# First loads on two queues, the first pair's scores in whole fp32, and the order of the attention's drain, in a fused attention, feed-forward and routed-experts kernel

## The chip, the cores and the metric

The kernel runs on one core of one Trainium2 chip. The metric is the device time of one execution in microseconds (us); the median of several runs is compared.

## The reference

Three stages follow one another, and only the first and the beginning of the second are touched here.

```
attention, q, k, v: (4, 8, 576, 64)
    scores = q @ k^T / 8, block-causal mask (blocks of 64), softmax, @ v
feed-forward, x: (2304, 512), w_in: (512, 2048), w_out: (2048, 512)
    h = x @ w_in;  g = h if h > 0 else exp(h) - 1;  x = g @ w_out
experts, 8 of them, top one of a gate, rows with x @ w_skip > 0
    out = x + gate * (relu(x @ w1[e]) @ w2[e])
```

## The kernel before

The 32 heads are worked on as 16 pairs: the two heads of a pair have 64 columns each, and lie side by side on the 128 partitions. A pair's step on TensorE holds the scores of five row blocks (`scores(n, i, u)`, u = 0 to 4, into the PSUM tile `s_ps`), the transposes of the softmax's rows (`turn_pair`, `turn_head`, `turn_last`, `turn_corner`, into `t_ps`), the transposes of the next pair's q and k (`prep`, groups g = 0, 1, 2 of 4, 1 and 4 transposes), and the products with v (`values`, into `o_ps`). The pairs are software pipelined: while pair n is scored, pair n - 1 is turned and pair n - 2's products with v end. The order on each engine is written out by hand in `step`, and the engines meet only at semaphores.

All large products are made in three passes of a rounded type: each operand is split in a high and a low half (`qk_hi`, `qk_lo`; `wi_hi`, `wi_lo`; `xt_hi`, `xt_lo`; `wo_hi`, `wo_lo`), and high x high, low x high and high x low are added up. The scores of block u = 0 alone are made from the unsplit `qk_f` in plain fp32 (L587). ScalarE copies q and k out of PSUM into `qk_f` (`prep_copy`, L493 to L500); GpSimd splits them for the pairs 1 to 15, VectorE for pair 0 (L437, L439).

SyncE issues every plain load and store, in one queue. At the start it issues q, k of pair 0, q, k of pair 1, v of both, and so on, three DMAs each (L228 twice, L230). For each pair it also stores the 9 x 128 reciprocals of the row sums to DRAM (L250), loads them back spread over the partitions (`load_recips`, L257 and L260, four DMAs), and stores the pair's result, `attn_sb`, to `attn_t` (`store`, L244). VectorE multiplies the result by the spread reciprocals (`final`, L424) before that store.

The drain is what follows the last pair's step. TensorE turns block 3 of pair 15, ends pair 14's products, makes `hidden(0)` (the feed-forward's first h chunk, 12 matmuls with 384 columns), turns the reciprocals into `t_ps`, waits until ScalarE has copied them out, turns the last block, makes `hidden(1)` and then pair 15's products with v. After that the feed-forward's steps begin: `ff_hidden(0, f)`, 12 matmuls, and two chunks behind it `ff_output(0, f - 2)`, 9 matmuls with 512 columns. The output product of chunk f needs chunk f of w_out in both halves: SyncE loads it (L1048, 256 KB, into one of four buffers, waiting until GpSimd has made the low half of the chunk four before), ScalarE makes the high half (`wo_high`, L1576), GpSimd the low half (L1166). ScalarE's steps are in program order: `wo_high(f + 2)`, `exp(0, f)`, `g_hi(0, f - 1)`. GpSimd, after the low half of chunk 3, waits for the store of all pairs' results and writes constants (L1109 to L1125) before it makes the low half of chunk 4. The chunks 0 to 3 of w_out are loaded ahead of the last reciprocals, chunk 4 behind the last store, the others behind the loads of the next x block:

```
for f in range(WR, FC):
    load_wo(f)
    if f == WR:
        for stored in attend["stored"]:
            sp.wait_ge(stored, 16 * attend["pairs"] // 2)
        load_x(1)
        load_gates()
```

## Time and profile before

| | |
|---|---|
| Median of 3 runs | 828.46 us (827.02 to 831.72) |
| The profiled execution's own time | 828.58 us |
| Its span, first to last instruction | 826.8 us |
| TensorE matmuls busy | 797.1 us, 96% of the span |
| VectorE, ScalarE, GpSimd busy | 530.1, 341.4, 244.9 us |
| Attention and its drain | from the start to about 203 us |
| Feed-forward | to about 640 us, experts after it |

Times are read from the start of the span. "PEld" is TensorE's weight load, "SPq" the issuing of a DMA on SyncE, and the bracket at the end of a row of the timeline is the engine's idle time just before the instruction and what ended it. A matmul's row begins when it begins; rows overlap, since matmuls are pipelined.

### The profile page before, as it was taken

To read this page: it belongs to the slowest core of one execution; us is meant where nothing else is said; L and a number is where in the kernel's file an instruction comes from. 1 tells how busy PE (TensorE), PEld (TensorE's weight loads), DVE (VectorE), ACT (ScalarE), POOL (GpSimd) and SP (SyncE) were. 2 spreads that over 40 slices of the span, in tenths; PEclk is the share of its full clock that TensorE was granted. 3 is DMA by queue.
4 is the path that set the end of the run, shared out by engine and by line. 5 is a ranking of instruction groups with operands and counts; after the bars stand their busy time and mean duration, and the time that the engine had idled before them with its cause. 6 is when DMAs were issued, how large, how long until landed. Compare 5 with 4: busy or idle time off the path is not lost.

```text
span 826.8 us, 14738 instructions
## 1 busy us (share of the span) xinstructions
PE 797.1 (96%) x4618; PEld 663.0 (80%) x4619; DVE 530.1 (64%) x1294; ACT 341.4 (41%) x831; POOL 244.9 (30%) x240
## 2 busy tenths in 40 slices
PE   5999999999999999999999999999997999999995
PEld 3777777777889988888888898889875777887884
DVE  3777778775433587488478658734765799267342
ACT  3666666563442322222322232232443676256141
POOL 2667766675351021021012002000012313123111
PEclk9999999999999999999999999999998999999998
DMA  6355556644424201200110020050341799264000
GB/s 141 99 145 155 158 155 155 169 134 144 116 65 160 86 20 61 77 21 20 64 32 20 1 77 7 20 204 3 126 161 31 236 324 366 81 223 148 20 27 8
DMA packets 102912, 88.09 MB, mean 107 GB/s; under 512 B 66676, under 2 KB 78340, under 8 KB 102736
## 3 DMA queue, kind: packets, MB, share of 16 engines
q1 hardware_dynamic: 99808, 82.48, 32.4%
q0 software_dynamic: 3056, 5.00, 1.8%
q8 instruction: 26, 0.43, 0.2%
q14 instruction: 22, 0.18, 0.1%
HBM read 72.26 MB, written 18.34 MB: 110 GB/s over the span
## 4 chain that ended last, share of the span: by engine, by line
PE 74%; SPq 12%; DMA 4%; issue 4%; DVE 3%; ACT 1%; DVEq 1%; POOL 0%; POOLq 0%; ACTq 0%
PE h_ps L1686 11%; PE out_ps L1686 11%; PE h_ps L1687 11%; PE h_ps L1688 11%; PE out_ps L1688 11%; PE out_ps L1687 11%; SPq L228 4%; SPq L230 3%; DMA recip_rows<-r_rows 3%; SPq L260 2%; SPq L257 2%; PE t_ps L600 1%; PE o_ps L650 1%; PE out_ps L1822 1%; PE s_ps L592 1%
## 5 line engine op out<-in xcount | busy, mean ns | idle before, releaser
L1513 ACT ACTIVATE ex<-h_ps 128x384 f32<-128x384 f32 x96 | 47.1, 491 | 269.1 <-PE h_ps L1688 268.5
L1686 PE MATMUL h_ps<-xt_hi,wi_hi 128*128 128x384 f32 x384 | 131.9, 343 | 0.0
L1687 PE MATMUL h_ps<-xt_lo,wi_hi 128*128 128x384 f32 x384 | 129.9, 338 | 0.0
L1688 PE MATMUL h_ps<-xt_hi,wi_lo 128*128 128x384 f32 x384 | 129.9, 338 | 0.0
L1352 DVE TENSOR_SCALAR ex<-ex 128x384 f32<-128x384 f32 x96 | 36.9, 384 | 143.3 <-ACT ex L1513 142.2
L1686 PE MATMUL out_ps<-wo_hi,gt 128*128 128x512 f32 x288 | 114.8, 398 | 1.8 <-DVE gt L1345 1.8
L1688 PE MATMUL out_ps<-wo_hi,gt 128*128 128x512 f32 x288 | 114.0, 396 | 0.0
L1687 PE MATMUL out_ps<-wo_lo,gt 128*128 128x512 f32 x288 | 113.4, 394 | 0.0
L512 ACT ACTIVATE prob<-s_ps,negmax 128x128 f32<-128x128 f32 (+2 forms) x144 | 77.8, 548 | 63.9 <-DVE negmax L379 57.9
L1234 DVE CUSTOM_DVE_ANT_0 x2t<-x,w_raw 128x512 bf16<-128x512 f32 x108 | 82.8, 808 | 0.4
L1130 POOL TENSOR_TENSOR xt_lo<-x_raw,xt_hi 128x384 fp32r<-128x384 f32 x20 | 28.4, 1419 | 163.0 <-ACT xt_hi L1528 162.9
L1686 PEld LDWEIGHTS h_ps<-xt_hi,wi_hi 128*128 128x128 f32 x384 | 72.3, 188 | 3.4
L1687 PEld LDWEIGHTS h_ps<-xt_lo,wi_hi 128*128 128x128 f32 x384 | 72.3, 188 | 3.1
L1138 POOL DMA_INDIRECT route_table<-entry,slot x18 | 21.0, 1165 | 177.2 <-DVE slot L1313 160.9
L1688 PEld LDWEIGHTS h_ps<-xt_hi,wi_lo 128*128 128x128 f32 x384 | 72.2, 188 | 0.0
L379 DVE TENSOR_REDUCE negmax<-s_ps 128x2 f32<-128x256 f32 (+1 forms) x64 | 51.3, 823 | 21.5 <-PE s_ps L595 21.5
L1688 PEld LDWEIGHTS out_ps<-wo_hi,gt 128*128 128x128 f32 x288 | 54.2, 188 | 13.3
L1686 PEld LDWEIGHTS out_ps<-wo_hi,gt 128*128 128x128 f32 x288 | 54.1, 188 | 11.4 <-issue 2.4
L1687 PEld LDWEIGHTS out_ps<-wo_lo,gt 128*128 128x128 f32 x288 | 54.1, 188 | 8.8
L600 PE MATMUL t_ps<-ident,prob 128*128 128x128 f32 (+1 forms) x400 | 58.5, 284 | 1.6 <-DVE pt L403 0.7
L1355 DVE TENSOR_TENSOR ex<-h_ps,ex 128x384 f32<-128x384 f32 x96 | 53.5, 558 | 3.3
L600 PEld LDWEIGHTS t_ps<-ident,prob 128*128 128x128 f32 (+1 forms) x400 | 43.5, 141 | 13.8 <-issue 11.3
(174 smaller groups left out, 1629.8 us busy)
## 6 DMA issues: line engine op xcount, KB each, us to landing
w_raw<-in_moe_w_dram SPq DMA_DIRECT2D x56, 512.0 KB, 5.2
attn_t<-attn_sb SPq DMA_DIRECT2D x16, 288.0 KB, 2.2
x_raw<-attn_t SPq DMA_DIRECT2D x24, 192.0 KB, 2.4
out_dram<-x SPq DMA_DIRECT2D x18, 256.0 KB, 2.1
x_rows<-x SPq DMA_DIRECT2D x18, 256.0 KB, 2.5
raw_qk<-in_q_dram SPq DMA_DIRECT2D x32, 128.0 KB, 2.4
raw_qk<-in_k_dram SPq DMA_DIRECT2D x32, 128.0 KB, 2.4
v<-in_v_dram SPq DMA_DIRECT2D x32, 128.0 KB, 2.6
```

What stands on the lines that cost most here:

```text
L228: sp.dma_start(dst[:, 0:FULL, h, :], heads[h, 0:FULL * P, :] .rearrange("(t p) d -> p t d", p=P)).then_inc(landed, 16)
L379: dve.tensor_reduce(heads_cols(negmax, u), s_pair(u), AX_X, ALU.max, negate=True).then_inc(max_done, 1)
L512: act.activation(dst, src, ACT.Exp, bias=negmax[:, c:c + 1], accum_out=rowsum[i][:, c:c + 1]).then_inc(exp_done, 1)
L600: return pe.transpose(t_ps[0:src.shape[1], bank, at:at + P], src, ident[:, :])
L1130: pool.tensor_tensor(xtk(b % 2, 1, k), x_raw[k][:, :], xtk(b % 2, 0, k).bitcast(F32), ALU.subtract).then_inc(x_lo_done, 1)
L1234: ins = dve.tensor_tensor_reduce(dot_rows[:, ((E + 1) * t + e) % 2], x2[s][:, :], all_skip if e == E else all_gates[:, e, :], 1.0, 0.0, AL ...
L1352: dve.tensor_scalar(e, e, 1.0, -1.0, ALU.min, ALU.add).then_inc(em_done, 1)
L1355: dve.tensor_tensor(e, h_ps[:, f % 2, 0:NB], e, ALU.max).then_inc(g_done, 1)
L1513: act.activation(ex[:, f % 2], h_ps[:, f % 2, 0:NB], ACT.Exp).then_inc(ex_done, 1)
L1686: pe.matmul(dst, stat[0], mov[0], start=start, stop=False, skip_group_check=True)
L1687: pe.matmul(dst, stat[0], mov[1], start=False, stop=False, skip_group_check=True)
L1688: return pe.matmul(dst, stat[1], mov[0], start=False, stop=stop, skip_group_check=True)
```

## The change

Five edits:

- The loads of k for the pairs 0 and 1 are issued on ScalarE's queue, at its very beginning; those of q stay on SyncE's.
- Pair 0's three groups of transposes go to three PSUM banks (two of `t_ps`, one of `o_ps`) without a wait between them. VectorE copies the third group out, in place of ScalarE, and no longer splits pair 0.
- Pair 0's scores are made from the unsplit `qk_f` in plain fp32 in all five blocks.
- In the drain, `hidden(0)` comes before the turns of block 3; the last block and the corner are turned before the reciprocals, and these go to a free place in `s_ps` (`last_rows`). The turn of the last block waits for VectorE's copy of block 3 in place of ScalarE's copy of the reciprocals.
- Chunks 4 to 7 of w_out are issued after the last reciprocals' loads and ahead of the last store; the loads of the next x block and of the gates follow that store.

```
+    def load_q(eng, n, i):
+        load(eng, q, n, raw[i][:, 0], raw_tail[i][0:TAIL], qk_in[i])
+    def load_k(eng, n, i):
+        load(eng, k, n, raw[i][:, 1], raw_tail[i][TAIL:P], qk_in[i])
...
-        load_qk(0, 0)
-        load_qk(1, 1)
+        for i in range(2):
+            load_q(sp, i, i)
         load_v(0, 0)
...
-        load_wo()
+        first_wo()
         store_recips(PAIRS - 1, 1)
         store(PAIRS - 2, 0)
         load_recips(PAIRS - 1, 1)
+        next_wo()
         store(PAIRS - 1, 1)
...
-                pool.wait_ge(split_hi, 2 * n + part + 1)
+                pool.wait_ge(split_hi, 2 * (n - 1) + part + 1)
...
-        for part, (a, b) in enumerate(((Q, K), (K, QK))):
-            dve.wait_ge(prep_out, (1, 3)[part])
-            dve.tensor_copy(qk_hi[0][:, a:b], qk_f[0][:, a:b]).then_inc(split_hi, 1)
-            dve.wait_ge(split_hi, part + 1)
-            dve.tensor_tensor(qk_lo[0][:, a:b], qk_f[0][:, a:b], qk_hi[0][:, a:b].bitcast(F32),
-                              ALU.subtract).then_inc(split_lo, 1)
+        dve.wait_ge(prep_t, 3)
+        dve.tensor_copy(qk_f[0][:, K:K + FULL * P], o_ps[:, 0:BANK]).then_inc(split_lo, 2)
...
-        for g in range(3):
-            prep_copy(0, 0, g, (0, 1, 0)[g])
+        for i in range(2):
+            load_k(act, i, i)
+        for g in range(2):
+            prep_copy(0, 0, g, g)
...
+            whole = isinstance(n, int) and n == 0
             if u == 0:
                 wait(pe, exp_done, exps(n - 1, 3, 1))
                 wait(pe, split_lo, 2 * n + 2)
+                if whole:
+                    pe.wait_ge(prep_out, 3)
...
+                    if whole:
+                        last = pe.matmul(dst, qk_f[i][:, Q4:QK], qk_f[i][:, keys], start=True, stop=True)
+                        continue
...
-            if u == 0:
+            if u == 0 or whole:
...
         for g in range(3):
-            if g == 2:
-                pe.wait_ge(prep_out, 1)
-            prep(0, 0, g, (0, 1, 0)[g])
+            prep_into(0, 0, g, t_ps[:, g] if g < 2 else o_ps[:, 0:BANK])
...
+        pe.wait_ge(wi_lo_done, PAIRS)
+        pe.wait_ge(exp_done, exps(last[0], 3, 1))
+        hidden(0)
         for h in range(2):
             turn_head(last[0], 3, h)
         values(*older, 1)
-        pe.wait_ge(wi_lo_done, PAIRS)
-        hidden(0)
-        pe.wait_ge(turned, turns(last[0], 3, 1))
+        turn_last(last[0], turned, turns(last[0], 3, 1))
+        turn_corner(last[0])
         pe.wait_ge(rec_done, PAIRS)
-        turn_recips(last[0])
-        turn_last(last[0])
-        turn_corner(last[0])
+        turn_recips(last_rows)
         hidden(1)
...
-            attend["sync"](sp, first_wo)
-            for f in range(WR, FC):
+            attend["sync"](sp, first_wo, next_wo)
+            for stored in attend["stored"]:
+                sp.wait_ge(stored, 16 * attend["pairs"] // 2)
+            load_x(1)
+            load_gates()
+            for f in range(2 * WR, FC):
                 load_wo(f)
```

## Rows read from the trace of the kernel before

**Rows 1.** The page, the chain that ended last, shares by engine

```profile
PE 74%; SPq 12%; DMA 4%; issue 4%; DVE 3%; ACT 1%; DVEq 1%; POOL 0%; POOLq 0%; ACTq 0%
```

**Rows 2.** Busy time in a stretch (us, count) of PE, PEld, DVE, ACT, POOL; clock; DMA share; GB/s

```profile
68.20:79.40 11.20, 11.20 (x103) 8.21 (x99) 8.78 (x17) 7.22 (x25) 7.60 (x7) 1.00 0.60 156
```

**Rows 3.** The chain that ended last, the first loads: start, us, what

```profile
0.87 0.45 SPq L228
...
3.89 2.42 DMA raw_tail<-in_k_dram
```

**Rows 4.** Busy time in a stretch, columns as in Rows 2, first loads

```profile
2.00:4.00 2.00, 0.00 (x0) 0.00 (x0) 0.06 (x1) 1.28 (x1) 0.15 (x2) 1.00 0.65 148
```

**Rows 5.** Timeline of the start, PE, ACT: start, us, engine, line, what, idle before

```profile
2.23 1.28 ACT L493 ACT_TABLE_LOAD   x1 [2.08 <-POOL qk_f L318]
...
6.45 1.08 PE L559 MATMUL t_ps<-ident,raw_qk 128*128 128x128 f32 x4 [6.45 <-DMA raw_tail<-in_k_dram]
...
7.32 0.42 PE L559 MATMUL t_ps<-ident,raw_tail 128*128 128x128 f32 x1
...
11.50 0.80 PE L587 MATMUL s_ps<-qk_f 64*128 64x128 f32 x4 [2.17 <-DVE qk_lo L439]
...
12.09 0.27 PE L595 MATMUL s_ps<-mask_row,half_row 64*128 64x64 bf16 x2
```

**Rows 6.** The page, the costliest groups: a DMA issued by another engine than SyncE

```profile
L1138 POOL DMA_INDIRECT route_table<-entry,slot x18 | 21.0, 1165 | 177.2 <-DVE slot L1313 160.9
```

**Rows 7.** Timeline, pair 0's step and the beginning of pair 1's, PE

```profile
16.59 1.12 PE L559 MATMUL t_ps<-ident,raw_qk 128*128 128x128 f32 x4 [0.76 <-ACT qk_f L493]
...
18.23 0.63 PE L592 MATMUL s_ps<-qk_hi,qk_lo 64*128 64x512 f32 x2
...
18.66 0.63 PE L592 MATMUL s_ps<-qk_lo,qk_hi 64*128 64x512 f32 x2
...
23.23 0.49 PE L587 MATMUL s_ps<-qk_f 64*128 64x128 f32 x4
```

**Rows 8.** The line L424 on VectorE: what it waited for (us, times)

```profile
  DMA r_sb<-recip_rows: 2.4, 1
```

**Rows 9.** Timeline of the drain, POOL, PE, DVE, SP

```profile
191.25 0.99 POOL L358 TENSOR_TENSOR xt_lo<-x_raw,xt_hi 128x384 fp32r<-128x384 f32 x1
...
192.13 1.09 PE L600 MATMUL t_ps<-ident,prob 128*128 128x128 f32 x8 [0.41 <-DVE pt L397]
...
196.51 0.27 PE L600 MATMUL t_ps<-ident,recip 128*9 128x128 f32 x1
...
197.23 0.74 PE L600 MATMUL t_ps<-ident,prob 128*128 128x128 f32 x5 [0.45 <-ACT r_rows L525]
...
197.89 0.69 DVE L403 COPY pt<-t_ps 128x512 f32<-128x512 f32 x1 [2.73 <-PE t_ps L600]
...
200.13 0.60 SPq L260 DMA_DIRECT2D r_sb<-recip_rows  x1
...
202.96 0.76 DVE L424 TENSOR_TENSOR attn_sb<-o_ps,r_sb 128x576 f32<-128x576 f32 x1 [0.92 <-PE o_ps L650]
```

**Rows 10.** DMA issues from 185 to 240: count, KB each, median us to landing

```profile
w_raw<-in_moe_w_out_dram SPq DMA_DIRECT2D x15, 256.0 KB, 3.1
...
r_sb<-recip_rows SPq DMA_DIRECT2D x4, 16.0 KB, 2.7
```

**Rows 11.** Timeline of the feed-forward's first steps, SP, ACT, POOL, PE

```profile
203.75 0.34 SPq L244 DMA_DIRECT2D attn_t<-attn_sb  x1
...
206.87 0.63 ACT L1576 ACTIVATE wo_hi<-w_raw 128x512 fp32r<-128x512 f32 x1 [5.87 <-DMA w_raw<-in_moe_w_out_dram]
...
207.81 1.29 POOL L1166 TENSOR_TENSOR wo_lo<-w_raw,wo_hi 128x512 fp32r<-128x512 f32 x1
...
210.52 0.47 PE L1686 MATMUL out_ps<-wo_hi,gt 128*128 128x512 f32 x1 [1.11 <-DVE gt L1345]
...
215.61 0.47 PE L1686 MATMUL out_ps<-wo_hi,gt 128*128 128x512 f32 x1 [0.66 <-DVE gt L1345]
```

More of the change, by code:

```diff
@@ L221, in heads_cols, with load, sync @@
         return t[:, 0:2 * FULL].rearrange("p (h u) -> p h u", h=2)[:, :, u]
[L223 to L230 removed]
+    last_rows = s_ps[0:COLS, 2 * BANK:2 * BANK + P]
+    def load(eng, t, n, dst, tail, landed):
+        heads = t.rearrange("b h s d -> (b h) s d")[bass.ds(2 * n, 2)]
+        for h in range(2):
+            eng.dma_start(dst[:, 0:FULL, h, :], heads[h, 0:FULL * P, :]
+                          .rearrange("(t p) d -> p t d", p=P)).then_inc(landed, 16)
+        eng.dma_start(tail, heads[:, FULL * P:S, :].rearrange("h s d -> s h d")).then_inc(landed, 16)
+    def load_q(eng, n, i):
+        load(eng, q, n, raw[i][:, 0], raw_tail[i][0:TAIL], qk_in[i])
+    def load_k(eng, n, i):
+        load(eng, k, n, raw[i][:, 1], raw_tail[i][TAIL:P], qk_in[i])
+    def sync(sp, first_wo, next_wo):
         def load_qk(n, i):
             wait(sp, prep_t, 3 * (n - 1))
[L235 to L236 removed]
+            load_q(sp, n, i)
+            load_k(sp, n, i)
         def load_v(n, i):
             wait(sp, pv_done, n - 1)
[L240 removed]
+            load(sp, v, n, vb[i], vb[i][0:TAIL, FULL, :, :], v_in[i])
         def store(n, i):
@@ L500, in prep_copy @@
                 act.activation(qk_f[i][:, K + FULL * P:Q4], src[:, TAIL:P], ACT.Copy)\
-                   .then_inc(prep_out, 1)
+                   .then_inc(prep_out, 2 if isinstance(n, int) and n == 0 else 1)
         def exp(n, i, u):
@@ L538, in step @@
             if past:
-                recip_rows(past[0])
+                recip_rows(past[0], t_ps[0:COLS, 1, R0:R0 + P])
             if now:
@@ L549, in scalar, with prep_into @@
         wo_high()
-        recip_rows(PAIRS - 1)
+        recip_rows(PAIRS - 1, last_rows)
     def tensor(pe, hidden):
         def prep(n, i, g, bank):
+            prep_into(n, i, g, t_ps[:, bank])
+        def prep_into(n, i, g, dst):
             if g == 0:
@@ L558, in prep @@
             for c, tile in enumerate(tiles):
-                last = pe.transpose(t_ps[:, bank, c * P:(c + 1) * P],
+                last = pe.transpose(dst[:, c * P:(c + 1) * P],
                                     tile.rearrange("p h d -> p (h d)"), ident[:, :])
@@ L626, in turn_head, with turn_last @@
             last.then_inc(pt_done, 1)
-        def turn_last(n):
+        def turn_last(n, ready, value):
             wait(pe, exp_done, exps(n, LAST, 0))
-            wait(pe, r_row_done, n + 1)
+            wait(pe, ready, value)
             for j in range(FULL):
@@ L638, in turn_corner, with turn_recips @@
             turn(0, 2 * P, prob4[:, FULL * P:S]).then_inc(pt_done, 1)
-        def turn_recips(n):
-            turn(1, R0, recip[:, :]).then_inc(r_turned, 1)
+        def turn_recips(dst):
+            pe.transpose(dst, recip[:, :], ident[:, :]).then_inc(r_turned, 1)
         def values(n, i, part):
@@ L681, in step @@
             if past:
-                turn_recips(past[0])
+                turn_recips(t_ps[0:COLS, 1, R0:R0 + P])
             if now:
@@ L688, in step @@
             if past:
-                turn_last(past[0])
+                turn_last(past[0], r_row_done, past[0] + 1)
             if now:
@@ L1053, in first_wo, with next_wo @@
                     load_wo(f)
-            attend["sync"](sp, first_wo)
-            for f in range(WR, FC):
-                load_wo(f)
-                if f == WR:
-                    for stored in attend["stored"]:
-                        sp.wait_ge(stored, 16 * attend["pairs"] // 2)
-                    load_x(1)
-                    load_gates()
+            def next_wo():
+                for f in range(WR, 2 * WR):
+                    load_wo(f)
+            attend["sync"](sp, first_wo, next_wo)
[4 more added lines that the diff above has]
+            for f in range(2 * WR, FC):
+                load_wo(f)
             broadcast_gates()
```

14 lines of the change are left out of this document (2 added, 12 removed).

## The prediction

> **What bounds the kernel now.** I read the page first, for the chain of work that ended last: three quarters of it are TensorE [rows 1]. Then I cut the attention into stretches of one pair, 11.2 us each: TensorE is busy for all 11.20 us of such a stretch, the next engine, VectorE, for 8.78 [rows 2]. So between the first pair and the drain nothing but TensorE's own work sets the pace, and a shift of the first scores passes through whole. SyncE's queue runs close behind it: once, at the last pairs but a few, VectorE waited 2.4 us for the spread reciprocals [rows 8]. That queue starts its work on a pair when the reciprocals of the pair before are ready, so it moves with TensorE, and this wait stays as it is. What is left to win lies at both ends of the attention: before the first scores at 11.50 [rows 5], and from 190 to 216, where TensorE stands still four times, for 0.41, 0.45, 1.11 and 0.66 us [rows 9, 11].
>
> **Before the first transposes.** Six DMAs bring q and k of pair 0. SyncE begins the first at 0.87 and the sixth at 3.89, which is 0.60 us for each, and the sixth lands 2.42 later, at 6.31 [rows 3]. TensorE starts at 6.45. With k on ScalarE's queue the third DMA of either queue is issued when the third is now, at about 1.9, and if nothing else counted it would land at 1.9 + 2.4 = 4.3: a gain of 2.0. But the transfers share the DMA engines. From 2 to 4 us they are busy for 0.65 and move 148 GB/s [rows 4], so full they would move 228. q and k of pair 0 are 2 x 288 KB = 590 kB, or 2.6 us at that rate. Started at 2.0 as now, they end at 4.6, and now the last landing follows the end of the moving (590 kB at 148 GB/s from 2.0, 5.9) by 0.4. That gives 5.0, and 5.2 with a little of pair 1's loads among them. I take 5.2, a gain of 1.1; the bounds are 2.0 and nothing (6.31, if the queues only took turns). The Trainium skill, DMA: Bandwidth & Descriptors, section Issuing engines are not separate DMA queues, says that DMAs of several issuing engines run on the same 16 DMA engines and interleave, and that a second issuer saves sequencer time alone. That speaks against the gain of 2.0, and the share of 0.65 lets the queue's time be saved only up to the free third; by the rule with no such headroom the sum would be 1.1 smaller.
>
> **Up to the first scores.** Now TensorE makes five transposes, waits until ScalarE has emptied a bank, makes four more; ScalarE copies; VectorE splits; the scores start 11.50 - 6.45 = 5.05 after the first transpose. After the change nine transposes follow each other at (7.32 - 6.45) / 4 = 0.22 us and the last ends 8 x 0.22 + 0.42 = 2.2 after the first [rows 5]. VectorE's copy of 512 columns out of PSUM takes 0.69 as at L403 [rows 9]. 2.2 + 0.7 + two handovers of 0.03 make 2.95: a gain of 2.1, and the scores start at 5.3 + 2.95 = 8.25 in place of 11.50, 3.25 earlier. The cover that this needs is ScalarE: its six issues, at SyncE's 0.60 each, last from 0.87 to 4.5, its table load of 1.28 [rows 5] to 5.8, the copies of two groups (some 1.3) then wait for TensorE and end at about 7.7, half a microsecond ahead of VectorE. The trace has no DMA issued by ScalarE. The nearest row of another engine is GpSimd's indirect DMA, 1165 ns [rows 6]; six of these would end at 7.9, the table load at 9.15, the copies at 10.45, and of the 3.25 only 1.0 would be left. SyncE's own price is the nearer one, since the DMA is the same. The Trainium skill, ScalarE: Activation LUTs, section What ACT_TABLE_LOAD costs, counts 2.66 us for a switch of tables, with a drain behind the load. By that ScalarE would end at 8.5 and the first part of the sum be 0.3 smaller; the row shows 1.28, with the first copy four us behind it, so it cannot say.
>
> **Pair 0 in whole fp32.** The row of block 0 prices it: both heads, 128 columns, fp32, occupy TensorE from 11.50 to 12.09 [rows 5], 0.59, of which 0.43 are four passes of 128 columns at 1.2 GHz. A pass of the rounded type with 512 columns takes 18.66 - 18.23 = 0.43 [rows 7], one pass at 1.2 GHz. So fp32 is four passes against three, and the heads still run side by side. One pass more costs 0.21 (block 1, 256 columns), 0.32 (384), 0.43 (512) and 0.48 (last block, 576). Block 1's and those of blocks 3 and 4 lie on the path; block 2's 0.32 goes into the 0.76 for which TensorE waits for ScalarE at 16.59 [rows 7]. Sum 1.1 lost. At worst the two heads run one after the other, which would cost 0.85, 1.3 and 1.7 more in blocks 1 to 3; 0.59 is less than the 0.85 which two heads in turn would need in block 0, so this is out. VectorE's splits in pair 0 go, and GpSimd's first split has its slack as now, since it starts from ScalarE's copy.
>
> **The clock.** In this stretch the trace's granted clock reads 1.00 [rows 4], yet matmuls run at 1.2 GHz: the same four fp32 matmuls take 0.80 at 11.50 and 0.49 at 23.23 [rows 5, 7]. The rise to 2.4 GHz comes shortly before 23, after TensorE has been at work without a stop since 16.6. If it comes at the same place in the work, it costs nothing. If it comes at the same time, 2.1 us more of work run at half speed, and 1.05 are lost. If fp32 keeps the array busier and the rise comes 5 us earlier in the work, up to 2.5 are won. I take nothing, between the two.
> Start: 3.25 - 1.1 = 2.1 us.
>
> **The drain.** All times here are those of before, without the shift. TensorE now waits at 191.7 for VectorE's copy of a transpose, 0.41, until 192.13. `hidden(0)` fits there: what it waits for is there, the last low half of x at 192.24 [rows 9], needed by its last quarter alone at 193.2, and w_in's halves, which GpSimd made before it. Behind that wait stand all of the drain's instructions, so it matters, but its cover is 1 us. Then everything follows without a pause: the wait of 0.45 for ScalarE's reciprocal rows goes too, since the last block is turned first. Pair 15's products end at 202.93 - 0.41 - 0.45 = 202.05 or so. The reciprocals are turned at 196.7 in place of 196.51 [rows 9], so their last load is issued at 200.3 in place of 200.13, and lands 2.7 later [rows 10], at 203.0: VectorE's product of pair 15, now at 202.96 and released by TensorE, starts at 203.1 and waits for this DMA. That costs nothing by itself.
>
> The next step is where the gain is. SyncE issues w_out's chunk 4 at 201.0, not after the store at 203.75, and chunks 5 to 7 by 203; the store follows at 204. Chunk 4 lands 3.1 later [rows 10], at 204.1, while ScalarE now stands idle for 5.87 until 206.87 for it [rows 11] with the feed-forward's exp behind it. With the products over at 202.05, `hidden(2)` ends at 204.2, exp and the two halves of g are ready at about 206.7, and the output product that needs them is reached at 202.05 + 2.1 + 2.1 + 2.1 = 208.4 without the wait of 1.11. The next one, which waits 0.66 at 215.61 since chunk 5 comes behind the x loads, is reached at 212.6. So the drain gives 215.6 - 212.6 = 3.0 us: 0.41 + 0.45, 1.11 + 0.66, and 0.3 for three smaller gaps in the same stretch. The store waits behind 1 MB of w_out on the DMA engines and lands perhaps 1 us later; GpSimd's low half of chunk 4, now at 207.81 [rows 11] behind that store, then comes at 208.5 or 209, and TensorE needs it only at the fifth output product, at about 221. If this cover were gone, each microsecond of the store's would be one of TensorE's.
>
> **Sum.** 828.58 (the profiled execution; 826.8 of span and 1.8 around it) - 2.1 - 3.0 = 823.5. The median is 0.12 below that execution, so I predict 823.4 us.
>
> **The rivals.**
> The start gives little: ScalarE's issues cost like GpSimd's 1.17 [rows 6], the scores start at about 10.5, the start gives 1.0 - 1.1 = nothing. Then only the drain is left, 825.5. For it: no row shows such an issue. Against: the same kind of DMA costs 0.60 on SyncE.
> The second queue moves nothing sooner (the rule above, as a mechanism here: the DMA engines, busy for 0.65, cannot be filled further, so q and k land at 6.3): 1.1 less, 824.5.
> The clock rises earlier in the work, since whole fp32 streams more columns: 1 to 2.5 more, 821 to 822.4.
> The drain's gain is given back: chunks 4 to 7 crowd the store and the reciprocals' loads; VectorE's last product comes 2 us late, and with it g of chunk 2, so the 1.77 of waits stay: 825.2.
> Slower than before: ScalarE's queue. If each of its six issues takes 2.5 us, they end at 15.9, and with the table load and the copies the scores start at 18.5, 7.0 late; with 1.1 of fp32 lost and 3.0 won in the drain this is 5.1 more, 833.7. It decides from 1.7 us an issue on, where start and drain cancel (scores at 13.4). No row is that dear, but none shows such an issue either.
> That nothing comes of either end would need a wait behind the attention that absorbs them; the chain [rows 1] shows TensorE there, and I give it no chance of its own.
>
> **Chances.** Forecast, 3.9 to 6 us faster: 0.52. Clock earlier: 0.16. Start gives little or nothing, or queue without effect: 0.18. Drain given back: 0.10. Slower: 0.04. The forecast's own range is 822.4 to 824.5. A change of 0.5%, 4.1 us, is about what a measurement of this kernel tells from none (the three runs before span 4.7), so it parts at 824.3. The forecast lies only 1 us beyond that, so of its 0.52 I count 0.45 as faster, and with the clock's case 0.61; slower 0.04; the rest, 0.35, within. The range goes from the clock's far case to the drain given back and half of the start's: 820.8 to 826.0.
>
> **What would show it.** DMA landing of k's tail at 5.2; first transposes at 5.3, nine in a row; VectorE's copy; scores at about 8.3; four matmul passes of blocks 1 to 4; pair 1's first scores at 21.1 in place of 23.23. In the drain no wait of TensorE between block 3 and the third output product, VectorE's last product released by a DMA, ScalarE's high half of chunk 4 without its 5.9 of idle. Wrong it would be if ScalarE's copies ended after VectorE's, if the rise of the clock stayed at 22 to 23, or if the store's delay reached GpSimd's constants by more than 10 us.

## The result, and the profile after

| | before | after |
|---|---|---|
| Median | 827.98 us (7 runs, 825.82 to 831.72) | 822.27 us (7 runs, 821.41 to 823.22) |
| Ratio after / before, 95% interval | | 0.9929 [0.9909, 0.9949] |
| The profiled execution | 828.58 us | 823.07 us |
| Its span | 826.8 us | 821.0 us |

The change makes the kernel faster by 0.7%, 5.7 us; 823.4 was predicted. The measured 822.27 lies 0.1 outside the forecast's own range (822.4 to 824.5), in that of the rival "the clock rises earlier" (821 to 822.4), and inside the whole range. Ratios here and below leave out a single execution, one of e3's, which took 1295 us. The chain by engine has shifted as the removed waits would have it: TensorE's share is up from 74% [rows 1].

```profile
PE 77%; SPq 10%; issue 4%; DMA 3%; DVE 3%; ACT 1%; DVEq 1%; ACTq 0%; POOL 0%; POOLq 0%
```

**Where the time went.** Five moments cut both spans. The differences are taken from the starts of the same instructions in the two timelines.

| moment | before | after | won in the stretch that ends here |
|---|---|---|---|
| pair 0's first scores | 11.50 | 9.28 | 2.22 |
| pair 1's first scores | 23.23 | 20.60 | 0.41 |
| pair 15's first scores | 181.08 | 177.67 | 0.78 |
| output product of chunk 3 | 219.91 | 212.85 | 3.65 |
| end of the span | 826.77 | 821.00 | -1.29 |

Sum 5.77, against a forecast of 5.15 (3.25, -1.1, nothing, 3.0, nothing, in the order of the table). The five stretches are off by -1.03, +1.51, +0.78, +0.65 and -1.29: errors of 5.3 us in all, of which 0.6 is left because they have both signs. That the total came out so near is in good part luck.

The start, the chain that ended last, first loads (start, us, what); it answers to [rows 3]:

```profile
2.01 4.13 DMA raw_tail<-in_k_dram
```

and busy time in stretches, columns as in [rows 4]:

```profile
2.00:4.00 2.00, 0.00 (x0) 0.00 (x0) 0.06 (x1) 0.00 (x0) 0.15 (x2) 1.00 1.02 231
4.00:6.00 2.00, 0.00 (x0) 0.00 (x0) 0.00 (x0) 1.06 (x1) 0.00 (x0) 1.00 1.32 220
1.00:6.40 5.40, 0.13 (x1) 0.16 (x2) 0.93 (x8) 1.28 (x1) 0.91 (x7) 1.00 0.97 183
```

The last piece of pair 0's k is now issued at 2.01, not at 3.89 [rows 3], but takes 4.13 us to land, not 2.42: it lands at 6.14, against 6.31. The DMA engines do move more: 231 GB/s where it was 148 [rows 4], just what the prediction took for full (228), at a busy share of 1.02. But from 1 to 6.4 us they move 183 GB/s x 5.4 us = 990 kB, and pair 0's q and k are 590. The rest is pair 1's and v's, which the two queues also issue earlier.

The start, timeline of ACT, DVE and PE, answering to [rows 5] and [rows 7]:

```profile
0.88 1.10 ACTq L229 DMA_DIRECT2D raw_qk<-in_k_dram  x2
2.01 0.71 ACTq L231 DMA_DIRECT2D raw_tail<-in_k_dram  x1
2.76 1.38 ACTq L229 DMA_DIRECT2D raw_qk<-in_k_dram  x2
4.17 0.68 ACTq L231 DMA_DIRECT2D raw_tail<-in_k_dram  x1
4.94 1.28 ACT L500 ACT_TABLE_LOAD   x1 [4.78 <-issue]
...
8.34 0.22 ACT L508 ACTIVATE qk_f<-t_ps 128x64 f32<-128x64 f32 x1
```

```profile
8.54 0.69 DVE L447 COPY qk_f<-o_ps 128x512 f32<-128x512 f32 x1 [6.48 <-PE o_ps L573]
```

```profile
6.27 1.09 PE L573 MATMUL t_ps<-ident,raw_qk 128*128 128x128 f32 x4 [6.27 <-DMA raw_tail<-in_k_dram]
...
9.28 0.80 PE L607 MATMUL s_ps<-qk_f 64*128 64x128 f32 x4 [0.86 <-DVE qk_f L447]
...
14.56 1.12 PE L573 MATMUL t_ps<-ident,raw_qk 128*128 128x128 f32 x4 [0.46 <-ACT qk_f L500]
15.60 2.08 PE L607 MATMUL s_ps<-qk_f 64*128 64x512 f32 x4
17.47 0.26 PE L615 MATMUL s_ps<-mask_row,half_row 64*128 64x64 bf16 x2
17.66 1.38 PE L620 MATMUL t_ps<-ident,prob 128*128 128x128 f32 x6
...
19.85 0.82 PE L620 MATMUL t_ps<-ident,prob 128*128 128x128 f32 x6
20.60 0.49 PE L607 MATMUL s_ps<-qk_f 64*128 64x128 f32 x4
```

ScalarE's six issues last 3.87 us together, 0.65 each. Its copies end at 8.56, VectorE's at 9.23: ScalarE is ahead, and releases nothing. Six transposes of the same kind take 1.38 us at 17.66 and 0.82 at 19.85: the step to 2.4 GHz comes between them. In the kernel before it comes shortly ahead of 23.23 [rows 7].

The drain, timeline of PE, DVE, SP, ACT and POOL, answering to [rows 9] and [rows 11]:

```profile
188.04 0.42 PE L1707 MATMUL h_ps<-xt_hi,wi_hi 128*128 128x384 f32 x1
...
190.21 1.03 PE L620 MATMUL t_ps<-ident,prob 128*128 128x128 f32 x8
...
204.46 0.40 PE L1707 MATMUL out_ps<-wo_hi,gt 128*128 128x512 f32 x1
```

```profile
199.92 0.76 DVE L434 TENSOR_TENSOR attn_sb<-o_ps,r_sb 128x576 f32<-128x576 f32 x1 [2.19 <-DMA r_sb<-recip_rows]
```

```profile
197.58 2.00 SPq L1066 DMA_DIRECT2D w_raw<-in_moe_w_out_dram  x4
200.71 0.34 SPq L252 DMA_DIRECT2D attn_t<-attn_sb  x1
```

```profile
204.47 0.34 POOL L1130 MEMSET x<- 128x288 int32 x1 [7.15 <-DMA attn_t<-attn_sb]
...
206.28 1.59 POOL L1187 TENSOR_TENSOR wo_lo<-w_raw,wo_hi 128x512 fp32r<-128x512 f32 x1
```

No row of TensorE carries a bracket here any more. VectorE's last product is released by the reciprocals' DMA, as forecast, and the last store lands 3.4 us after its issue ended; GpSimd's low half of chunk 4 starts at 206.28, with TensorE's need of it at 217.04.

### The profile page after: what moved, and what is told of

Its sections match the earlier page's. It is cut to its first block, busy times and chain, and to the rows that moved or that the text cites. A ratio compares the mean times of both kernels' runs of the same rounds, so it can differ in the third digit from the quotient of the medians.

```text
span 821.0 us, 14719 instructions
## 1 busy us (share of the span) xinstructions
PE 796.7 (97%) x4610; PEld 661.8 (81%) x4611; DVE 527.3 (64%) x1291; ACT 341.0 (42%) x830; POOL 244.3 (30%) x240
## 4 chain that ended last, share of the span: by engine, by line
PE 77%; SPq 10%; issue 4%; DMA 3%; DVE 3%; ACT 1%; DVEq 1%; ACTq 0%; POOL 0%; POOLq 0%
PE h_ps L1707 12%; PE out_ps L1707 11%; PE h_ps L1708 11%; PE h_ps L1709 11%; PE out_ps L1709 11%; PE out_ps L1708 11%; SPq L229 4%; SPq L231 3%; DMA recip_rows<-r_rows 2%; PE o_ps L670 2%; PE t_ps L620 2%; SPq L268 2%; SPq L265 2%; PE out_ps L1843 1%; PE s_ps L612 1%
## 5 line engine op out<-in xcount | busy, mean ns | idle before, releaser
L389 DVE TENSOR_REDUCE negmax<-s_ps 128x2 f32<-128x256 f32 (+1 forms) x64 | 51.3, 822 | 21.3 <-PE s_ps L615 21.3
L1707 PE MATMUL out_ps<-wo_hi,ht_hi 128*128 128x512 f32 x120 | 50.9, 424 | 3.7 <-DVE ht_lo L1442 3.5
```

Source lines behind the costliest of these rows:

```text
L389: dve.tensor_reduce(heads_cols(negmax, u), s_pair(u), AX_X, ALU.max, negate=True).then_inc(max_done, 1)
L1707: pe.matmul(dst, stat[0], mov[0], start=start, stop=False, skip_group_check=True)
```

## The experiments

The kernel before was run again beside each group of kernels, and each ratio is to those runs of it (medians 827.21 beside e1, e2, e4 and e7; 827.65 beside e3, e5 and e6; 828.15 beside e8 to e10; 828.31 beside e11 and e12). So kernels of different groups are compared by their ratios. The landmarks of all profiles, in us, as differences between the starts of the same instructions; the last column is the mean granted clock from 610 to 650 us.

| kernel | median | ratio [95%] | first scores | to pair 1 | to pair 15 | to out. prod. 3 | to the end | clock |
|---|---|---|---|---|---|---|---|---|
| before | 827.98 | | 11.50 | 11.73 | 157.85 | 38.83 | 606.86 | 0.91 |
| after | 822.27 | 0.9929 [0.9909, 0.9949] | 9.28 | 11.32 | 157.07 | 35.18 | 608.15 | 0.87 |
| e1 | 822.39 | 0.9938 [0.9924, 0.9951] | 9.32 | 10.91 | 157.49 | 35.19 | 607.95 | 0.91 |
| e11 | 822.30 | 0.9923 [0.9901, 0.9946] | 9.02 | 10.90 | 156.98 | 35.21 | 606.98 | 0.91 |
| e4 | 823.48 | 0.9950 [0.9937, 0.9964] | 11.09 | 11.00 | 157.76 | 35.20 | 608.12 | 0.87 |
| e2 | 825.25 | 0.9979 [0.9970, 0.9988] | 8.91 | 11.66 | 156.95 | 39.06 | 608.20 | 0.87 |
| e3 | 824.66 | 0.9953 [0.9936, 0.9971] | 11.50 | 11.88 | 156.86 | 35.18 | 606.99 | 0.91 |
| e5 | 828.54 | 1.0014 [0.9997, 1.0030] | 11.32 | 10.76 | 158.20 | 39.09 | 607.03 | 0.91 |
| e6 | 825.15 | 0.9965 [0.9950, 0.9979] | 11.44 | 10.76 | 157.12 | 36.52 | 606.97 | 0.91 |
| e7 | 820.15 | 0.9911 [0.9896, 0.9926] | 8.45 | 10.14 | 157.16 | 35.20 | 608.16 | 0.87 |
| e8 | 821.13 | 0.9916 [0.9902, 0.9930] | 8.29 | 10.06 | 157.90 | 35.19 | 607.80 | 0.91 |
| e9 | 820.77 | 0.9907 [0.9891, 0.9922] | 9.14 | 11.69 | 158.51 | 35.20 | 605.95 | 1.00 |
| e10 | 819.57 | 0.9895 [0.9880, 0.9910] | 8.10 | 10.05 | 160.20 | 35.19 | 605.98 | 1.00 |
| e12 | 820.00 | 0.9896 [0.9873, 0.9919] | 8.29 | 10.06 | 157.70 | 35.19 | 606.00 | 1.00 |

**e1_k_on_sync: the second queue undone.**

```
         for i in range(2):
             load_q(sp, i, i)
+            load_k(sp, i, i)
...
-        for i in range(2):
-            load_k(act, i, i)
```

> The changed kernel with one edit undone: k of the pairs 0 and 1 goes back to SyncE's queue, behind the q of both. In the changed kernel the third DMA of k was issued at 2.01 but took 4.13 to land, at 6.14, against 6.31 before the change. Theory A, the shared DMA engines are the limit: q and k of pair 0 land no earlier with two queues. Here k of pair 0 is issued behind q of pair 1, so its tail is issued at about 5.7 and lands at 8.1; the first transposes start at 8.2 in place of 6.27, everything after is 1.9 later, some 824.2. If q and k of a pair were issued in turn it would be 6.4, as before the change. Theory B, ScalarE's issues delay its copies (they end at 8.56, as late as VectorE's copy begins): with the six issues gone, the table load comes at 2.2 and ScalarE's copies end 0.1 to 0.3 sooner after the transposes; the scores still wait for VectorE's copy.

The kernel that ran issues q, k of pair 0 and then q, k of pair 1 in turn, so of the expectation its last case holds. Timeline, PE:

```profile
6.31 1.09 PE L572 MATMUL t_ps<-ident,raw_qk 128*128 128x128 f32 x4 [6.31 <-DMA raw_tail<-in_k_dram]
...
14.60 0.67 PE L572 MATMUL t_ps<-ident,raw_qk 128*128 128x128 f32 x4 [0.46 <-ACT qk_f L501]
...
20.23 0.49 PE L606 MATMUL s_ps<-qk_f 64*128 64x128 f32 x4 [1.02 <-POOL qk_lo L340]
```

With one queue the transposes start at 6.31, with two at 6.27. Over the profiles whose chain shows it, the last piece of pair 0's k lands at 6.31, 6.17, 6.30, 6.12 and 6.24 with one queue (before, e1, e3, e5, e6) and at 6.14, 5.76, 5.91 and 5.99 with two (after, e2, e4, e9): on the mean the second queue is worth 0.3 us. The other two rows show something else. Up to 14.6 this profile is that of the changed kernel shifted by 0.04, but here the four transposes take 0.67, there 1.12: the clock has risen 3 to 5 us earlier behind the same work. Most of that is lost again, since GpSimd's split of pair 1 is then not ready, and TensorE waits 1.02 for it.

**e11_k1_sync: only pair 0's k on ScalarE's queue, pair 1's behind its q on SyncE's.**

```
         for i in range(2):
             load_q(sp, i, i)
+            if i == 1:
+                load_k(sp, i, i)
...
-        for i in range(2):
-            load_k(act, i, i)
+        load_k(act, 0, 0)
```

> The changed kernel, but k of pair 1 is back on SyncE's queue, behind q of pair 1; ScalarE issues the three loads of k of pair 0 alone. In the changed kernel the DMA engines moved 231 GB/s from 2 to 4 us and 183 GB/s from 1 to 6.4 us, that is 990 kB, of which pair 0's q and k are 590: the rest is pair 1's and v's. Theory (the last tile of pair 0's k landed at 6.14 instead of 5.2 because loads that nobody needs yet share the engines): with three loads fewer in flight it lands at 5.0 to 5.4, the first transposes start at 5.1 to 5.5 and the first scores 3.0 later, at 8.1 to 8.5, and pair 1's q and k, issued by 6.3 and landed by 8.8, are still in time for their transposes at 10.0; the time is 0.5 to 1.0 less than 822.3. Rival (a load issued by ScalarE lands late whatever else is moving): 6.1, scores at 9.2, no change.

The chain that ended last, and busy time in a stretch:

```profile
2.00 3.88 DMA raw_tail<-in_k_dram
```

```profile
1.00:6.40 5.40, 0.39 (x2) 0.42 (x3) 0.93 (x8) 1.28 (x1) 0.91 (x7) 1.00 0.93 182
```

5.88 in place of 6.14, and the median is the same. The theory's 5.0 to 5.4 did not come. Nor do the 0.26 show an effect: with the changed kernel's own loads e2 landed at 5.76. As many bytes were moved as in the changed kernel (182 against 183 GB/s), since pair 1's loads come on through SyncE's queue. So this kernel did not take away what it was to take away, and that the sharing is the whole cause of the late landing stays argued. A kernel in which pair 1's loads wait for pair 0's landing was not tried.

**e4_pair0_split: pair 0 in three passes of the split operands again.** Loads, banks and drain stay as changed.

```
-        dve.tensor_copy(qk_f[0][:, K:K + FULL * P], o_ps[:, 0:BANK]).then_inc(split_lo, 2)
+        dve.wait_ge(prep_out, 1)
+        dve.tensor_copy(qk_hi[0][:, Q:K], qk_f[0][:, Q:K]).then_inc(split_hi, 1)
...
+        dve.tensor_copy(qk_f[0][:, K:K + FULL * P], o_ps[:, 0:BANK]).then_inc(copied, 1)
...
+        dve.tensor_copy(qk_hi[0][:, K:QK], qk_f[0][:, K:QK]).then_inc(split_hi, 1)
...
-            whole = isinstance(n, int) and n == 0
+            whole = False
```

> The changed kernel with whole fp32 undone: pair 0 in three passes of the rounded type, so VectorE splits pair 0 again, partly after its copy. Loads, banks and the drain stay. Theory A (the clock's rise depends on how much TensorE streams): the first scores start at about 11.1 in place of 9.28, the rise to 2.4 GHz comes at 22 to 23 as before the change and not at 18.9, and pair 1's scores at about 22.8, 2.2 later than in the changed kernel; 824.3. Theory B (the rise comes by the time since the engine began): the rise is at 18.9 or so here too, pair 1's scores start at about 21.3, 0.7 later; 823.0.

```profile
6.04 1.09 PE L585 MATMUL t_ps<-ident,raw_qk 128*128 128x128 f32 x4 [6.04 <-DMA raw_tail<-in_k_dram]
...
11.09 0.80 PE L617 MATMUL s_ps<-qk_f 64*128 64x128 f32 x4 [2.90 <-DVE qk_lo L458]
```

From the first transposes to the first scores 5.05 us, as before the change (5.05), against 3.01 with whole fp32: while VectorE splits, the three banks give nothing. The 2.04 come of leaving out the split with the banks in place. A kernel without the split and with the old banks was not run; an estimate from the trace of before, where ScalarE's last copy releases VectorE at 10.00, 3.55 after the first transpose, gives 1.5 to the split and the other 0.5 to the banks and VectorE's copy. Whole fp32 then has the dearer passes; over the run e1, with whole fp32 and one queue, has a median 1.1 us below e4's, with intervals that overlap. Of the two theories on the clock neither came as written: pair 1's scores start at 22.09, between 21.3 and 22.8, and products of the last block take 0.44 at 20.46 and 0.30 at 20.94, so the clock rose there.

**e2_start_only and e3_drain_only: each end by itself.** e2 is the changed kernel with the drain's order and w_out's loads of before; e3 is the kernel before with the changed drain.

From the changed kernel to e2 (the loads' part):

```
-            attend["sync"](sp, first_wo, next_wo)
-            for stored in attend["stored"]:
...
-            for f in range(2 * WR, FC):
+            attend["sync"](sp, first_wo, lambda: None)
+            for f in range(WR, FC):
                 load_wo(f)
+                if f == WR:
```

From the kernel before to e3:

```
-        turn_recips(last[0])
-        turn_last(last[0])
-        turn_corner(last[0])
+        turn_recips(last_rows)
         hidden(1)
...
         load_recips(PAIRS - 1, 1)
+        next_wo()
         store(PAIRS - 1, 1)
```

> The changed kernel with both edits of the drain undone: the old order of TensorE there, and w_out's chunks 4 to 7 loaded as before. My sum: the start alone is 2.6 by the trace (pair 1's scores at 20.60 in place of 23.23), so about 825.3, with TensorE's waits of 0.41, 0.45, 1.11 and 0.66 back. Rival, the start's gain is taken up by SyncE's queue in the attention: 827 to 828. Of the 0.8 that the changed kernel won between pair 1 and the drain, this run shows whether it belongs to the start (then block 3 of pair 15 is 3.4 earlier here too) or is a landing's luck (2.6).

> The kernel before with the two edits of the drain and nothing of the start. My sum of the prediction: 3.0 less; by the trace of the changed kernel 3.5 to 3.6 up to the fourth output product: 824.4 to 825, with pair 1's scores at 23.2 as before. Rival (the drain's gain is given back later, in the experts): the fourth output product 3.5 early, and the time within 1 of before, 827.

Start alone: ratio 0.9979, 1.7 to 2.0 us (by the ratio and by the medians). Drain alone: 0.9953, 3.0 to 3.9 us. Both: 0.9929, 5.7 to 5.9. They add up within that uncertainty. The 0.78 of the middle belong to neither: from pair 1's scores to pair 15's e3, with the old start, takes 156.86 and e2 156.95, but e5, with the old start too, 158.20 and e9, with the new one, 158.51. The drain's stretch, 38.83 us before, is 39.06 in e2 and 35.18 in e3, in every kernel with the changed drain 35.18 to 35.21.

**e5_order_only and e6_wo_only: the drain's two edits apart, both on the kernel before.** e5 has the new order on TensorE and the reciprocals in `last_rows`; e6 only the loads:

```
         load_recips(PAIRS - 1, 1)
+        next_wo()
         store(PAIRS - 1, 1)
```

> The kernel before with TensorE's new order in the drain alone; w_out's loads as before. My sum: the waits of 0.41 and 0.45 go, but the last store comes no earlier, since VectorE's last product now waits for the reciprocals, and chunk 4's load is issued behind that store. So TensorE arrives 0.9 early and waits as much longer for g at the second output product: gain 0 to 0.2, 827.8. Rival, each edit gives its own share: 0.9 less, 827.1.

> The kernel before with the w_out loads alone; TensorE's order in the drain as before. My sum: chunk 4 lands at about 204.2, before hidden(2) ends at 205.0, so the waits of 1.11 and 0.66 go: 1.8 to 2.1 less, 826. Rival (the store behind 1 MB of loads delays something): GpSimd's low half of chunk 4 comes at 209.5 in place of 207.8, and if that matters TensorE waits at the fifth output product.

Timeline of PE, e5, and then of SP, e5:

```profile
209.63 0.47 PE L1688 MATMUL out_ps<-wo_hi,gt 128*128 128x512 f32 x1 [2.38 <-DVE gt L1347]
...
215.12 0.47 PE L1688 MATMUL out_ps<-wo_hi,gt 128*128 128x512 f32 x1 [1.02 <-DVE gt L1347]
```

```profile
202.88 0.34 SPq L246 DMA_DIRECT2D attn_t<-attn_sb  x1
203.26 0.43 SPq L1050 DMA_DIRECT2D w_raw<-in_moe_w_out_dram  x1
```

The order alone takes the waits of 0.41 and 0.45 away and gets them back: its waits for g are 2.38 and 1.02 in place of 1.11 and 0.66 [rows 11], the stretch is 39.09 against 38.83, the ratio 1.0014. The date for chunk 4 is set elsewhere: it is issued behind the last store, and that waits for VectorE's last product, which needs the spread reciprocals and is no sooner for the new order (it starts 21.81 after pair 15's scores in e5, at 202.09, and 21.88 before). Counted from pair 15's first scores, chunk 4 is issued at 203.26 - 180.28 = 22.98 in e5 and at 204.13 - 181.08 = 23.05 before. With the loads moved ahead of the store (e6) the stretch falls by 2.31, a little more than the 1.8 to 2.1 expected, and the order on top of it by 1.34 more.

**e7_warm: nine fp32 products of the identity in front of the first transposes,** while TensorE waits for the loads. They write a part of `o_ps` that later products overwrite before it is read; nothing is left out.

```
+        for c in range(9):
+            pe.matmul(o_ps[:, BANK:BANK + P], ident[:, :], ident[:, :], start=True, stop=True)
         for g in range(3):
             prep_into(0, 0, g, t_ps[:, g] if g < 2 else o_ps[:, 0:BANK])
```

> The changed kernel with nine more matmuls (identity by identity, whole fp32, 128 columns, into a part of o_ps that later products overwrite) on TensorE before it waits for the first loads, at 2.2 to 6.1, where it stands idle. Theory A (the clock rises after TensorE has been busy for some time): the rise comes by 10 in place of 18.9, blocks 1 to 3 of pair 0 take half as long, and pair 1's scores start 2 to 3 us earlier, some being given back to waits for ScalarE and VectorE: 819.5 to 820.5. Theory B (transposes do not count or the gap at 8.4 to 9.3 resets it): no earlier rise, 822.3. If nine run past the landing at 6.14, the transposes start late by as much, at most 0.5.

```profile
2.30 4.18 PE L679 MATMUL o_ps<-ident 128*128 128x128 f32 x18 [2.30 <-POOL qk_f L328]
...
8.45 0.49 PE L607 MATMUL s_ps<-qk_f 64*128 64x128 f32 x4 [0.86 <-DVE qk_f L447]
...
12.87 0.66 PE L573 MATMUL t_ps<-ident,raw_qk 128*128 128x128 f32 x4 [1.78 <-ACT qk_f L500]
13.46 2.08 PE L607 MATMUL s_ps<-qk_f 64*128 64x512 f32 x4
```

The first scores take 0.49, not 0.80: the engine runs at 2.4 GHz from about 6.8 us on, so theory A holds. Block 3, behind a wait of 1.78, takes 2.08 again: the level has fallen. Pair 1's scores start at 18.59, 2.0 earlier than in the changed kernel, and the median is 820.15.

**e8_warm_fill: the waits of pair 0's step filled too,** with three products before the first scores and seven behind block 2's.

```
+        for c in range(3):
+            pe.matmul(o_ps[:, BANK:BANK + P], ident[:, :], ident[:, :], start=True, stop=True)
...
                 scores(*now, 2)
+            if now and not past:
+                for c in range(7):
+                    pe.matmul(o_ps[:, BANK:BANK + P], ident[:, :], ident[:, :], start=True, stop=True)
```

> The changed kernel with idle TensorE time of the start filled: nine fp32 128x128 products before the first transposes (as in the kernel with warm-up), three more before the first scores (0.86 us of waiting there) and seven behind block 2's scores, where TensorE waited 1.78 us for ScalarE's copy (L500) and the clock fell right after. They write a bank that nothing reads. Theory (the fall at 13.6 us came of that wait): the granted clock stays at the fast level from 6.8 us on, block 3's scores take about 1.15 us instead of 2.08 and the last block's 0.6 instead of 1.15, pair 1's scores start at about 17.5 to 17.9 us instead of 18.59 (GpSimd's split of pair 1 may hold them at the end of that), and the whole takes 0.5 to 1 us less than 820.15. Rival (the level falls whatever the engine does, or the fillers delay what stands behind them): block 3 stays slow, pair 1's scores at 18.6 us or later, 820.2 us or more.

```profile
13.30 1.13 PE L607 MATMUL s_ps<-qk_f 64*128 64x512 f32 x4
...
18.35 0.49 PE L607 MATMUL s_ps<-qk_f 64*128 64x128 f32 x4 [1.03 <-POOL qk_lo L339]
```

The theory holds for the clock (block 3 in 1.13 us, with no wait of TensorE before it) and not for the time: TensorE now waits 1.03 for GpSimd's split of pair 1, so 0.24 us is left of the gain (18.35 for 18.59), and the median, 821.13, is not below e7's.

**e9_experts_fill: products put in front of the three waits at the experts' start,** on the changed kernel.

```
+            def fill(count):
+                for c in range(count):
+                    pe.matmul(lg_ps[:, 0:P], ident[:, :], ident[:, :], start=True, stop=True)
...
                     turn_h(0, 1)
+                    fill(10)
                     output(0, 0, range(FCE))
+                    fill(5)
                     turn_x(1)
                     pe.wait_ge(route, ROUTED)
+                    fill(5)
```

> The changed kernel with fillers where TensorE waits at the start of the experts: ten fp32 128x128 products in the wait of 2.50 us for ht_lo, five in that of 1.27 us for x_now, five in that of 1.51 us for m_xt_lo; they write a bank that nothing reads then. The changed kernel has two stretches at the half clock there, 3.41 and 6.83 us, the kernel before 3.41 and 3.41. Theory (these waits bring the stretches, and the longer second one gave back about 1.25 us of the drain's gain): no fall of the clock between 600 and 640 us; of 10.24 us at half clock about 2.5 lie in waits, so some 7.7 us of products take half as long: 3.9 us less, 818.4 us; at least 1.25 us less than the changed kernel. Rival (what sets the time there is not TensorE's clock but the chain through VectorE and GpSimd): the clock stays up and the time changes by under 0.5 us. Second rival: the fillers delay the products behind them and the time is longer.

Busy time in stretches, columns as in [rows 2]; the kernel before, after, and e1:

```profile
626.00:632.00 6.00, 5.08 (x15) 4.10 (x16) 2.84 (x13) 2.84 (x4) 1.28 (x2) 0.72 0.08 24
636.00:642.00 6.00, 4.49 (x14) 3.52 (x14) 5.25 (x6) 0.60 (x1) 1.81 (x2) 0.72 0.32 100
```

```profile
618.00:625.00 7.00, 5.11 (x16) 4.13 (x17) 3.59 (x17) 3.80 (x5) 1.28 (x2) 0.76 0.09 22
628.00:638.00 10.00, 8.11 (x27) 6.35 (x28) 7.21 (x10) 1.19 (x2) 3.22 (x5) 0.66 0.50 161
```

```profile
618.00:627.00 9.00, 5.84 (x24) 4.43 (x24) 4.18 (x21) 3.85 (x5) 1.28 (x2) 1.00 0.13 40
627.00:637.00 10.00, 7.04 (x21) 5.40 (x22) 7.53 (x12) 1.20 (x2) 2.18 (x3) 0.66 0.37 114
```

And e9, the same and a row of its timeline, PE:

```profile
610.00:650.00 40.00, 37.42 (x201) 29.76 (x201) 26.73 (x100) 16.08 (x25) 9.26 (x13) 1.00 0.35 109
```

```profile
630.07 0.66 PE L1808 MATMUL tr_ps<-ident_f,x_now 128*128 128x128 f32 x4 [1.55 <-DVE x_now L1423]
```

A granted clock of 0.72 over 6 us is 2 x 6 x (1 - 0.72) = 3.4 us at 1.2 GHz. So the kernel before has two stretches of 3.4 us, the changed one 3.4 and then 6.8, e1 the second of 6.8 alone, and e9 none; and the time from output product 3 to the end is 606.86, 608.15, 607.95 and 605.95. That goes by the second stretch, in all fourteen profiles: with 6.8 us (after, e1, e2, e4, e7, e8) it is 607.80 to 608.20, with 3.4 us (before, e3, e5, e6, e11) 606.86 to 607.03, with none (e9, e10, e12) 605.95 to 606.00. The first stretch costs next to nothing: from the output product behind the first wait (619.89 in the changed kernel) to the transposes of `x_now` it takes 8.5 us in before, after, e1 and e9 alike, since a faster TensorE only waits longer for VectorE (1.27 in the changed kernel, 2.68 in e1). So the longer second stretch gave back the 1.29, and without any of it 2.2 us are won, not the 3.9 expected, which counted both stretches. The wait for `x_now` was not filled: 1.55 us of it are left in e9, and the clock stayed up all the same.

**e10_all_fill and e12_all: everything together.** e10 is e8's and e9's edits in one; e12 has e11's loads besides, with seven and two products in front:

```
+        load_k(act, 0, 0)
...
+        for c in range(7):
+            pe.matmul(o_ps[:, BANK:BANK + P], ident[:, :], ident[:, :], start=True, stop=True)
```

> Both together: the fillers of the start and those of the experts. If the two are independent the gains against the changed kernel (822.3 us) add: 2.1 for the warm-up, 0.5 to 1 for the fillers of the start, 3.9 for those of the experts, so 815.3 to 815.8 us. If the experts' clock isn't what sets the time there: 819.3 us.

> Everything that helped: the loads as in the kernel with pair 1's k on SyncE's queue, seven fp32 128x128 products before the first transposes, two before the first scores, seven behind block 2's scores, and the fillers at the experts' start. Against the kernel with all fillers (819.57 us): if the loads land earlier, the first scores come at about 7.3 instead of 8.10, but GpSimd's split of pair 1 (its wait was 1.03 us there) moves with them, so pair 1's scores start at about 17.4 instead of 18.15, and the time is 818.8 us; if the loads don't land earlier, 819.6.

819.57 and 820.00 us, the lowest medians here and not to be told apart, from each other or from e7's; both ratios are below the changed kernel's. The gains do not add up to the 815.5 that was expected: e8's fillers give nothing, e9's 2.2 instead of 3.9, and e10's profile loses 3.1 us in the middle of the attention (160.20 against 157.07). Timeline of e10, PE, and busy time in two stretches:

```profile
161.14 0.66 PE L620 MATMUL t_ps<-ident,prob 128*128 128x128 f32 x4 [1.45 <-DVE pt L413]
```

```profile
160.00:165.00 5.00, 3.77 (x20) 2.40 (x22) 3.99 (x7) 3.54 (x11) 3.40 (x3) 0.79 0.81 220
165.00:170.00 5.00, 5.00 (x46) 3.38 (x44) 2.75 (x6) 0.85 (x5) 1.26 (x1) 0.87 0.33 98
```

TensorE waits 1.45 us there, behind spread reciprocals that come late, and the granted clock then is down for 2 x 5 x (0.21 + 0.13) = 3.4 us, which costs up to 1.7: together the 3.1. No other profile has a fall of the clock between pair 1's first scores and the experts; e9, with a wait of 1.35 at the same place, has none. In e12 the loads land at 5.94, no sooner than in the other kernels with two queues, so its time is near the expectation's second case, 819.6.

## Why the prediction was right, point by point

**The second queue: a term that failed.** "I take 5.2, a gain of 1.1" measured 0.17 in the two profiles compared and 0.3 on the mean of those that show the landing. The headroom was there and was used (148 to 231 GB/s), but the estimate filled it with pair 0's 590 kB and only "a little of pair 1's loads", while 990 kB were moved by 6.4. The rival "the second queue moves nothing sooner" is nearer to what happened than the forecast, though not by its reason, that the engines cannot be filled beyond 0.65: they went to 1.02. By the Trainium skill, DMA: Bandwidth & Descriptors, section Issuing engines are not separate DMA queues, the transfers of several issuers interleave on the same 16 engines; the trace agrees (4.13 us to landing for 2.42, the share at 1.02 and 1.32). The sum has a slip besides: 590 kB at 148 GB/s from 2.0 end at 6.0, not at 5.9, so the landing follows by 0.3.

**ScalarE's price: right.** 0.65 an issue against 0.60 taken, and the rival's 1.17 or 2.5 did not come. Its copies end 0.67 ahead of VectorE's.

**From the first transpose to the first scores: right.** 3.01 against 2.95. e4 shows that the banks without leaving out the split give nothing.

**Whole fp32: its price right, the clock beside it taken at nothing.** Block 3 from its first pass to its mask: 1.87 (17.47 - 15.60) against 1.45 (19.09 - 17.64), 0.42 for a forecast 0.43; block 2's extra goes into the wait, 0.46 for 0.76 [rows 7]. But pair 0's step became 0.41 shorter, not 1.1 longer, and this is the largest error of the sum. From block 3's mask to pair 1's scores it takes 3.13, not 4.14. That stretch holds the last block's dearer passes as well, so here the clock gave 1.0 and what those cost; the sum had it at nothing, the rival "rises earlier" at 1 to 2.5. The 1.00 of [rows 4], which the prediction read for this stretch, is that of 2 to 4 us, and the first 1.2 GHz never show in that column. Whether fp32 brings the rise forward is not settled. With the old start pair 1's scores come 11.73, 11.88, 10.76 and 10.76 after pair 0's (before, e3, e5, e6; mean 11.28), with the new one 11.32, 10.91, 10.90, 11.66 and 11.69 (after, e1, e11, e2, e9; mean 11.30): the rise wanders by several microseconds between runs of the same work, and the means show neither the loss of 1.1 nor a gain. These numbers hide part of it, since in e1 and e11 TensorE waits 1.0 for GpSimd's split at their end. Estimated from the lengths of the rows in which it comes, the rise is at 12.9 to 19.4 us in the five profiles with whole fp32 and at 20.0 to 23.2 in the five without (before, e3, e5, e6, and e4 with its new banks). That leans to "earlier", but with whole fp32 the scores also start 2 us sooner than in the others, and the places in the work overlap. The start's total, 2.63 in the profiles and 1.7 to 2.0 over all runs of e2, is near the forecast 2.1 because the scores' shift was 1.03 too high and pair 0's step 1.51 too low (1.1 by the means): luck, not a sum that held.

**The drain: right, a little small.** 3.65 against 3.0. The same stretch, from the turn of block 2 to output product 3, is 29.07 us with 26.44 of TensorE before and 25.44 with 25.44 after:

```profile
190.84:219.91 29.07, 26.44 (x162) 22.28 (x161) 12.65 (x26) 9.50 (x22) 12.36 (x21) 1.00 0.46 143
```

```profile
187.41:212.85 25.44, 25.44 (x161) 22.39 (x160) 12.05 (x26) 9.53 (x22) 12.51 (x20) 1.00 0.56 171
```

The four waits are 2.63, as summed; the remaining 1.0 is shown as busy. It is about 0.25 for each wait: e5 has two waits, of 3.40 together, and is 3.9 longer than the unbroken 12.6 from output product 0 to 3; before has two of 1.77 and is 2.27 longer; and e6, which keeps the other two, of 0.86, is 1.34 longer than the changed kernel over the whole stretch. The term "0.3 for three smaller gaps" should have been 1.0. The text also gave 0.86 to the order and 1.77 to the loads as if each stood alone; e5 shows that the order alone gives nothing. "Drain given back" did not come: the last product waits 2.19 for its DMA, as said, the store lands late, as said, and about 9 us of cover hold.

**"This wait stays as it is": wrong.** The wait of [rows 8] is that of pair 11, counted from 0, and it moved. VectorE before and after:

```profile
163.26 0.76 DVE L424 TENSOR_TENSOR attn_sb<-o_ps,r_sb 128x576 f32<-128x576 f32 x1 [2.38 <-DMA r_sb<-recip_rows]
```

```profile
159.77 0.76 DVE L434 TENSOR_TENSOR attn_sb<-o_ps,r_sb 128x576 f32<-128x576 f32 x1 [1.54 <-DMA r_sb<-recip_rows]
```

TensorE, behind VectorE's next copy, then waits 0.68 before and not at all after. Before, the store of the reciprocals took 3.3 us until their reload could be issued, after, 2.35. e9 has the changed kernel's attention and is worse than before (VectorE waits 3.05, TensorE 1.35; the store took 2.77 and was issued 1.2 later than in the changed kernel), and e3, with the old start, has 1.45 and nothing: the difference is how late SyncE's queue and those small transfers are in a run, and no credit of the change.

**Behind the drain: not foreseen.** The prediction gave no chance to a wait behind the attention that absorbs a gain, since the chain [rows 1] shows TensorE there. 1.29 us came back at the experts' start, not by a wait but by TensorE's clock: the second stretch at 1.2 GHz is 6.8 us long in the changed kernel and 3.4 before (e9). The waits around it are nearly the same (2.50, 1.12 and 1.51 us before; 2.50, 1.27 and 1.51 after). Why the stretch is longer in one profile and shorter in another is open: e11, with the changed drain, has the short one, e2, with the old drain, the long one. So the 1.29 are no steady price of the change either.

## What to carry to other kernels

A second issuing queue brought the first tile 0.3 us of the 1.1 hoped for, with the loads of later tiles brought forward beside it; count the bytes that land before the one that is waited for, of all queues (that these bytes are the cause was not separated here). Before a producer's order is changed to remove a wait, follow the chain that dates its consumer: here that ran through the reciprocals, the store and the queue behind it, and only moving the load past the store made the order worth anything. Where TensorE must wait at the start, idle products in front of the real ones bought 2 us. Filling later waits helps only where TensorE sets the pace behind them: in e8 the gain ended at GpSimd's split, and at the experts' start the first slow stretch cost nothing because VectorE set the date.

## What the runs showed of the hardware

- The first matmuls run at 1.2 GHz: unaided, until somewhere from 12.9 to 23.2 us, a different place in runs whose work is the same. With nine idle products from 2.30 on, 2.4 GHz was there at 6.8. In this kernel's start a wait of 1.78 us was followed by the lower level, and with the wait filled it was not. At the experts' start two stretches at the lower level lie around waits of 2.5, 1.1 to 1.3 and 1.5; with the first and the third filled but for 0.3 and 0.4 us, and 1.55 us of the second left (e9), there was none. Inside the attention a fall followed a wait of 1.45 in e10 and none followed 1.35 in e9.
- In the drain each of four waits of TensorE cost about 0.25 us more than its idle time in the row, hidden in rows that read as busy.
- Two issuing queues raised the moved rate from 148 to 231 GB/s and the time from issue to landing of one load from 2.42 to 4.13 us.
- A whole fp32 product of both heads costs four passes against three, the heads still side by side: 0.42 more for 512 columns at 1.2 GHz.
